# Token-major attend products in a single-core mLSTM and mixture-of-experts kernel

## What is computed

```python
for t in range(S):
    m_new = np.maximum(f_gate[:, :, t] + m, i_gate[:, :, t])
    f_stab = np.exp(f_gate[:, :, t] + m - m_new)
    i_stab = np.exp(i_gate[:, :, t] - m_new)
    m = m_new
    C = f_stab * C + i_stab * outer(v_t, k_t)
    n = f_stab * n + i_stab * k_t
    h = C @ q_t
    y[t] = sigmoid(o_gate_t) * h / max(|n . q_t|, 1)
```

## Time and profile before

| what | value |
|---|---|
| median of 3 runs | 378.28 us (377.2 to 378.36) |
| the profiled execution | 376.49 us |
| its span | 374.7 us |
| PE busy | 366.7 us, 98% |
| VectorE, ScalarE, GpSimd busy | 64%, 61%, 22% |
| granted PE clock | 1.0 throughout |

### The profile page before, as it was taken

One profiled execution on the slowest core, in us unless ns is written; L12 is line 12 of the kernel. 1 busy time (PEld: TensorE's weight loads), 2 busy tenths in 40 slices (PEclk: granted clock), 3 DMA queues, 4 the chain that ended last, 5 costly groups with the idle time before them and its releaser, 6 DMA issues.

```text
span 374.7 us, 9643 instructions
## 1 busy us (share of the span) xinstructions
PE 366.7 (98%) x3502; PEld 309.6 (83%) x3502; DVE 239.0 (64%) x576; ACT 229.9 (61%) x468; POOL 81.4 (22%) x124
## 2 busy tenths in 40 slices
PE   8999999999999999999999999999999999999996
PEld 6688777778777775354899999999999999999996
DVE  8778688468767864423877655565565556556553
ACT  4677776757667763120877666576666566666652
POOL 6674665447446540000000000000000000000000
PEclk9999999999999999999999999999999999999999
DMA  2869999999988979999100010010010001001002
GB/s 79 247 185 295 263 262 294 251 225 277 256 232 267 282 245 339 362 295 344 67 1 2 18 54 1 3 70 0 0 70 0 0 0 70 0 0 70 2 0 70
DMA packets 28792, 51.49 MB, mean 137 GB/s; under 512 B 2980, under 2 KB 20228, under 8 KB 28756
## 3 DMA queue, kind: packets, MB, share of 16 engines
q1 hardware_dynamic: 25388, 40.08, 36.4%
q10 hardware_dynamic: 3368, 10.93, 10.4%
HBM read 46.59 MB, written 4.33 MB: 136 GB/s over the span
## 4 chain that ended last, share of the span: by engine, by line
PE 92%; DMA 2%; ACT 2%; SPq 1%; issue 1%; DVE 1%; POOL 0%; ACTq 0%; POOLq 0%
PE heads_banks L1346 8%; PE heads_banks L1348 8%; PE heads_banks L1347 7%; PE high_banks L1347 7%; PE high_banks L1346 7%; PE high_banks L1348 7%; PE low_banks L959 6%; PE low_banks L1326 6%; PE heads_banks L980 5%; PE heads_banks L973 3%; PE high_banks L995 3%; PE low_banks L1014 3%; PE low_banks L939 3%; PE low_banks L1246 2%; PE high_banks L1005 2%; PE low_banks L1036 2%
## 5 line engine op out<-in xcount | busy, mean ns | idle before, releaser
L876 ACT ACTIVATE relu_h<-low_banks 128x512 f32<-128x512 f32 x94 | 56.3, 599 | 59.6 <-PE low_banks L1326 59.2
L1760 DVE CAST sq_hi<-sq_h 128x512 fp32r<-128x512 f32 x94 | 40.2, 427 | 64.1 <-ACT sq_h L881 63.5
L1762 DVE TENSOR_TENSOR sq_lo<-sq_h,sq_hi 128x512 fp32r<-128x512 f32 x94 | 65.1, 692 | 3.2
L881 ACT ACTIVATE sq_h<-relu_h 128x512 f32<-128x512 f32 x94 | 59.4, 632 | 3.0
L1346 PE MATMUL heads_banks<-wo_hi,sq_hi 128*128 128x320 f32 x192 | 59.3, 309 | 0.2 <-DVE sq_lo L1748 0.2
L1347 PE MATMUL high_banks<-wo_lo,sq_hi 128*128 128x320 f32 x192 | 59.4, 310 | 0.0
L1348 PE MATMUL high_banks<-wo_hi,sq_lo 128*128 128x320 f32 x192 | 59.4, 310 | 0.0
L1346 PE MATMUL high_banks<-wo_hi,sq_hi 128*128 128x320 f32 x192 | 59.4, 309 | 0.0
L1348 PE MATMUL heads_banks<-wo_hi,sq_lo 128*128 128x320 f32 x192 | 59.3, 309 | 0.0
L1347 PE MATMUL heads_banks<-wo_lo,sq_hi 128*128 128x320 f32 x192 | 59.3, 309 | 0.0
L1392 DVE TENSOR_TENSOR att_w<-low_banks,att_w 128x512 f32<-128x512 f32 x48 | 30.9, 685 | 25.4 <-PE low_banks L959 25.4
(11 more groups left out here) (217 smaller groups left out, 562.3 us busy)
## 6 DMA issues: line engine op xcount, KB each, us to landing
w_sb<-in_w SPq DMA_DIRECT2D x8, 1280.0 KB, 12.4
w_a<-in_w ACTq DMA_DIRECT2D x16, 512.0 KB, 7.0
kv_in<-in_kv SPq DMA_DIRECT2D x24, 320.0 KB, 8.6
qk_in<-in_qk SPq DMA_DIRECT2D x24, 256.0 KB, 4.8
o_in<-in_o_gate SPq DMA_DIRECT2D x24, 160.0 KB, 8.5
out<-out_sb SPq DMA_DIRECT2D x5, 640.0 KB, 3.2
wo_raw<-in_w_out SPq DMA_DIRECT2D x4, 640.0 KB, 11.5
w_b<-in_w ACTq DMA_DIRECT2D x8, 256.0 KB, 8.7
```

Of the source, the lines that this page charges most:

```text
L876: act.activation(relu_h[:, slot], bank[slot][:, :], ACT.Relu).then_inc(relu_done, 1)
L881: act.activation(sq_h[:, slot], relu_h[:, slot], ACT.Square).then_inc(sq_done, 1)
L1760: dve.tensor_copy(sq_hi[:, slot], sq_h[:, slot]).then_inc(hi_done, 1)
L1762: dve.tensor_tensor(sq_lo[:, slot], sq_h[:, slot], sq_hi[:, slot].bitcast(F32), ALU.subtract).then_inc(lo_done, 1)
```

## The change

The operands of the attend products change places. In the values part the masked weights (128 by 128) are loaded as weights and the values with their column of ones (41 columns) move; in the carried part the faded queries of two heads (128 by 128) are weights and the carried state moves. The heads so come out with tokens on partitions. The carried state is kept in blocks of two heads (`[P, 2, HP, 2, D + 1]`): both heads of a place j share the product, with zeros where a head's partitions meet the other head's columns, so that one product of 82 columns serves two heads. Two banks take turns for the heads, where one held them feature by feature in two halves and another their transposes. `copy_heads` and `turn_heads` go, and their semaphores. VectorE reads the denominators and heads from the attend bank; it updates the carried state ahead of the denominators, with an add for each half of the partitions. One clearing of `v_one` goes, and the one of `carry` grows with its tile.

```diff
-            carry = sb("carry", [P, 2, HP, DP], stack=own)
-            carry_faded = sb("carry_faded", [P, HP, D + 1], stack=own)
-            headsT = sb("headsT", [P, 2, 2, L], stack=own)
+            carry = sb("carry", [P, 2, HP, 2, D + 1], stack=own)
+            carry_faded = sb("carry_faded", [P, HP, 2, D + 1], stack=own)
...
-        heads_ps = heads_banks[:, :, 0:2 * L].rearrange("p o (i t) -> p o i t", i=2)
-        turned_ps = turned_bank[:, :].rearrange("p (j a e) -> p j a e", j=HP, a=2)
+        heads_ps = [own[:, :].rearrange("p (j a e) -> p j a e", j=HP, a=2) for own in (heads_bank, odd_bank)]
...
+        def place_of(j):
+            return 2 * (j % 2) + j // 2
+
+        def own_blocks(tile, r):
+
+            halves = tile[DP * r:DP * (r + 1)].rearrange("p (i t) a e -> p i (t a) e", i=2)
+            return halves[:, :, (slice(0, 4, 3), slice(1, 3))[r]]
...
-            sp.wait_ge(carry_ready, (NC - 1) * B)
+            sp.wait_ge(carry_ready, 2 * (NC - 1) * B)
...
             def weigh_keys(b, c):
...
-                at_least(pool, heads_turned, step(b, c) - 1)
+                at_least(pool, state_added, carries(b, max(c - 1, 0)))
...
-            pool.memset(v_one[:, :, :, D + 1:DP], 0.0).then_inc(v_cleared, 1)
...
             def copy_v(b, c):
...
-                at_least(act, heads_turned, step(b, c) - 1)
+                at_least(act, heads, step(b, c) - 1)
+                if (b, c) == (0, 2):
+                    act.wait_ge(state_added, 1)
...
-            def copy_heads(b, c):
-                act.wait_ge(heads, step(b, c) + 1)
-                at_least(act, heads_turned, step(b, c))
-                act.activation(headsT[:, :, :, :], heads_ps, ACT.Copy).then_inc(heads_out, 1)
...
             def attend(b, c):
 
                 s = c % 2
-                at_least(pe, heads_out, step(b, c))
+                to = heads_ps[step(b, c) % 2]
+                at_least(pe, norm_step, 4 * (step(b, c) - 2) + 3)
                 if c > 0:
                     pe.wait_ge(q_scaled, rescales(b, c))
-                    pe.wait_ge(carry_ready, carries(b, c))
+                    pe.wait_ge(carry_ready, 2 * carries(b, c))
                     for j in range(HP):
-                        for r in range(2):
-                            rows, a = slice(DP * r, DP * (r + 1)), half_of(r, j)
-                            pe.matmul(heads_ps[DP * a:DP * (a + 1), j % 2, j // 2], carry[rows, (c - 1) % 2, j], q_fade[rows, s, j],
-                                      start=j < 2, stop=False, skip_group_check=True)
+                        pe.matmul(to[:, place_of(j), :, 0:D + 1], q_fade[:, s, j], carry[:, (c - 1) % 2, j],
+                                  start=j == 0, stop=False, skip_group_check=True)
                 pe.wait_ge(weights, step(b, c) + 1)
                 pe.wait_ge(v_ready, step(b, c) + 1)
                 for j in range(HP):
                     for r in range(2):
-                        h, a = HP * r + j, half_of(r, j)
-                        mm = pe.matmul(heads_ps[DP * a:DP * (a + 1), j % 2, j // 2], v_one[:, s, h], att_w[:, s, h],
-                                       start=c == 0 and j < 2, stop=True, skip_group_check=True)
+                        h = HP * r + j
+                        mm = pe.matmul(to[:, place_of(j), half_of(r, j), 0:D + 1], att_w[:, s, h], v_one[:, s, h, 0:D + 1],
+                                       start=c == 0 and h == 0, stop=True, skip_group_check=True)
                 mm.then_inc(heads, 1)
...
-            def turn_heads(b, c):
-                pe.wait_ge(heads_out, step(b, c) + 1)
-                at_least(pe, x_ready, step(b, c))
...
-                for j in range(HP):
-                    mm = pe.transpose(turned_bank[:, P * j:P * (j + 1)], headsT[:, j // 2, j % 2], ident)
-                mm.then_inc(heads_turned, 1)
...
             def update_carry(b, c):
-                dve.wait_ge(state_added, carries(b, c) + 1)
                 at_least(dve, heads, step(b, c))
+                fresh = state_ps[:, :, 0:D + 1].rearrange("p (i t) e -> p i t e", i=2)
...
                 dve.wait_ge(fade_ready, rescales(b, c))
-                whole = fade_b[:, fade_slot(b, c), :, L - 1].unsqueeze(2).broadcast_to([P, HP, D + 1])
-                dve.tensor_tensor(carry_faded[:, :, :], carry[:, (c - 1) % 2, :, 0:D + 1], whole, ALU.mult).then_inc(carry_half, 1)
+                dve.wait_ge(carry_ready, 2 * carries(b, c))
+                whole = fade_b[:, fade_slot(b, c), :, L - 1].unsqueeze(2).broadcast_to([P, HP, 2 * (D + 1)])
+                both = "p j a e -> p j (a e)"
+                dve.tensor_tensor(carry_faded.rearrange(both), carry[:, (c - 1) % 2].rearrange(both), whole, ALU.mult).then_inc(carry_half, 1)
                 dve.wait_ge(carry_half, (NC - 2) * b + c)
-                dve.tensor_tensor(carry[:, c % 2, :, 0:D + 1], carry_faded[:, :, :], state_ps[:, :, 0:D + 1], ALU.add)\
-                    .then_inc(carry_ready, 1)
+                dve.wait_ge(state_added, carries(b, c) + 1)
+                for r in range(2):
+                    dve.tensor_tensor(own_blocks(carry[:, c % 2], r), own_blocks(carry_faded, r), fresh[DP * r:DP * (r + 1)], ALU.add)\
+                        .then_inc(carry_ready, 1)
...
             def denominators(b, c):
 
                 n = step(b, c)
-                dve.wait_ge(heads_turned, n + 1)
+                own_heads = heads_ps[n % 2]
+                dve.wait_ge(heads, n + 1)
+                at_least(dve, x_ready, n)
...
             def vec_step(b, c, half, nxt=True, cur=True, prev=True, rb=None):
+                if cur and c < NC - 1:
+                    update_carry(b, c)
                 if prev:
                     denominators(*before(b, c))
-                if cur and c < NC - 1:
-                    update_carry(b, c)
```

More of the change, by code:

```diff
@@ L341, in build_program @@
         decay_bank, score_bank = bank[0:2], bank[2:4]
-        merge_bank, heads_bank, turned_bank, side_bank = bank[4], bank[5], bank[6], bank[7]
-        heads_ps = heads_banks[:, :, 0:2 * L].rearrange("p o (i t) -> p o i t", i=2)
-        turned_ps = turned_bank[:, :].rearrange("p (j a e) -> p j a e", j=HP, a=2)
+        merge_bank, heads_bank, odd_bank, side_bank = bank[4], bank[5], bank[6], bank[7]
+        heads_ps = [own[:, :].rearrange("p (j a e) -> p j a e", j=HP, a=2) for own in (heads_bank, odd_bank)]
         state_ps = side_bank[:, 0:HP * DP].rearrange("p (j e) -> p j e", j=HP)
@@ L352, in build_program @@
         last_turn = bank[3][:, 0:NC * NS].rearrange("p (c s) -> p c s", c=NC)
[L353 removed]
+        late_turn = merge_bank[:, 0:NC * NS].rearrange("p (c s) -> p c s", c=NC)
         turn_ps = side_bank[:, 0:NC * NS].rearrange("p (c s) -> p c s", c=NC)
@@ L781, in _ @@
             src_high(1)
-            act.wait_ge(v_cleared, 2)
+            act.wait_ge(v_cleared, 1)
             copy_v(0, 0)
@@ L793, in act_step @@
                     raise_keyw(1)
[L794 to L797, removed]
+                if cur and c < NC - 1:
+                    raise_fade(b, c + 1)
                 if rb is not None and c == NC - 1 and b < B - 1:
@@ L988, in add_state @@
                 pe.wait_ge(v_ready, step(b, c) + 1)
-                at_least(pe, carry_ready, carries(b, c))
+                at_least(pe, carry_ready, 2 * carries(b, c))
                 if rb is not None:
@@ L1141, in pe_step @@
                     if cur and c > 0:
-                        pe.wait_ge(carry_ready, carries(b, min(c + 1, NC - 1)))
+                        pe.wait_ge(carry_ready, 2 * carries(b, min(c + 1, NC - 1)))
                     route(rb, c, 1 - half)
@@ L1212, in _ @@
             for k in range(KC):
-                mm = pe.matmul(turned_bank[0:P if k < 2 else DP, QUAD * k:QUAD * (k + 1)], slot_acc[:, P * k:min(P * (k + 1), DM)],
+                mm = pe.matmul(odd_bank[0:P if k < 2 else DP, QUAD * k:QUAD * (k + 1)], slot_acc[:, P * k:min(P * (k + 1), DM)],
                                fold_scaled[:, :], start=k == 0, stop=True, skip_group_check=True)
-            mm = pe.matmul(turned_bank[DP:P, 2 * QUAD:KC * QUAD], slot_acc[:, DM - DP:DM], fold_scaled[:, :],
+            mm = pe.matmul(odd_bank[DP:P, 2 * QUAD:KC * QUAD], slot_acc[:, DM - DP:DM], fold_scaled[:, :],
                            start=False, stop=True, skip_group_check=True)
@@ L1408, in denominators @@
             def denominators(b, c):
                 n = step(b, c)
-                dve.wait_ge(heads_turned, n + 1)
+                own_heads = heads_ps[n % 2]
+                dve.wait_ge(heads, n + 1)
+                at_least(dve, x_ready, n)
                 dve.wait_ge(gate_ready, n + 1)
                 halves = "p (j a) -> p j a"
-                dve.tensor_scalar(norm_neg[:, :].rearrange(halves, a=2), turned_ps[:, :, :, D], -2.0, 2.0,
+                dve.tensor_scalar(norm_neg[:, :].rearrange(halves, a=2), own_heads[:, :, :, D], -2.0, 2.0,
@@ L1419, in denominators @@
```

(2 more changed lines are left out.)

13 lines of the change are left out of this document (3 added, 10 removed).

## The result

| what | before | after |
|---|---|---|
| median of the runs side by side | 378.32 us (377.2 to 378.67, 4 runs) | 444.3 us (439.36 to 454.32, 4 runs) |
| the profiled execution, its span | 376.49, 374.7 | 446.29, 444.6 |
| mean granted PE clock in that span | 1.0 | 0.869 |
| the expert products start at | 162.8 us | 232.6 us |

The changed kernel takes 1.1658 times as long, 95% interval [1.1581, 1.1736]. The forecast was 398 us, 393 to 402. The four runs of the changed kernel differ more than those of before, and in the order of their granted clock: 439.36 us at 0.887, 442.31 at 0.88, 446.29 at 0.869, 454.32 at 0.849.

What follows compares the result with a forecast made beforehand. PE's issue rate was taken as the bound. Terms 23.0 - 1.1 + 1.8 + 0.1 - 2.2 - 1.3 = +20.3 us on the profiled 376.49 gave 396.8, stated as 398 us for the median, 8-in-10 range 393 to 402.

Steps and rivals of the forecast that it cites:

- Rival A: Attend products: a record's pace follows the moving columns, not the weights, so faster, 367 us; 4%.
- Rival B: Attend products: with wide weights the next load waits for the stream, 24 records take 3.76 us, 420 us total; 2%.
- Rival D: Attention steps: a new wait of 0.3 us a step for the faded queries, some 7 us in all, 405 us; 6%.
- Attend groups at 2.77 us: Carried and values products: 24 records at 0.11 plus 0.13 turn, against 1.62 before; +1.15 in 20 steps, +23.0.
- the first chunks: Three first chunks of later batches, no carried part: 1.89 us where 1.30 pass now, +0.59 each, +1.8.
- Heads transposes in ordinary steps: Removing them saves only 0.20 us in each of 11 steps, as PE then waits for x's copy: -2.2.
- rival C: x's copy never waited for, or small waits hide behind attend; the transposes' full 10 us come back, 391 us; 5%.
- Where logits follow: Seven steps with router logits: of the transposes' 0.44 us some 0.26 is given back, 0.18 saved each, -1.3.
- Chunk 4, nothing saved: In chunk 4 no state product follows and the chain is bare already, so removing the heads transposes saves nothing.
- The rest costs nothing: VectorE, ScalarE, GpSimd and SP work changed outside PE's groups adds no time; x's readiness has 2 us of cover.
- Sum: All terms together: 23.0 - 1.1 + 1.8 + 0.1 - 2.2 - 1.3 = +20.3 us.

Runs made afterwards that it cites:

- e1_pad: Changed kernel with both moving operands of attend zero-padded, 64 columns instead of 41 (values) and 128 instead of 82 (carried): 397.74 us.
- e10_padv_bank: Changed kernel with x's transposes in a bank of their own and the values part padded to 64 moving columns: 393.78 us.
- e3_split: Changed kernel with each attend product issued twice, for tokens 0 to 63 and 64 to 127, side by side in two column halves: 382.58 us.
- e6_bank_pad: e3_split with x's transposes in the bank free during attention and the values part padded to 64 moving columns: 382.47 us.
- e7_order: e6_bank_pad with SyncE issuing chunk 4's loads of queries, keys and values ahead of phi and the wait for stored rows: 381.58 us.
- e1c_padc: Changed kernel with only the carried part padded, 128 moving columns instead of 82; the values part moves 41: 404.51 us.

## Why the prediction was wrong

**The step that failed** is one that was taken without a sum. The prediction read a granted clock of 1.0 in every slice and used durations of before for everything that the change doesn't touch. So it put the clock at nothing without a reason: those durations hold only while the clock stays where it was. In the changed kernel 116 us of the span pass at 1.2 GHz. Of the 69.9 us of growth, e1_pad's span (396.1, clock 1.0) puts 21.4 on the groups and waits, and leaves the other 48.5 to the clock. The runs of the changed kernel say the same by themselves: from the fastest (span 437.6, clock 0.887, so 98.9 us at 1.2 GHz) to the slowest (452.6, 0.849, 136.7 us) 37.8 us more at the low clock cost 15.0 us, 0.40 each; 98.9 x 0.40 = 39 off 439.4 leaves 400, and e1_pad measures 397.7. No rival had such a mechanism: A and B were about a record's pace, D about waits. The range ended 37 us below the fastest run.

**The other steps, at full clock:**

- Attend groups at 2.77 us: 2.81 measured, 2.70 where a transpose follows (2.68 forecast), 1.91 in the first chunks (1.89 forecast). Right; with the measured values the term is 8 x 1.19 + 12 x 1.08 = 22.5, where 23.0 - 1.1 = 21.9 was forecast.
- Rival A, moving columns set the pace: refuted by the same numbers, and by 64 columns taking no longer than 41. Rival B, a load waits for the stream: refuted by the padded kernel, 0.99 and 1.83 at 128 and 64 columns.
- Heads transposes in ordinary steps, 0.20 each: 1.95 became 1.74. Right, and rival C, that x's copy is never waited for, is refuted with it.
- Where logits follow, 0.18 each: wrong, 0. The reckoning let the first 8 logit records run while the rest waits, and the group behind end sooner; it ends as late as before, 2.03 both. That is 1.3 us too much saved.
- Chunk 4, nothing saved: 1.22 before and after. Right.
- Rival D, 0.3 us a step for faded queries: refuted. The padded kernel has one such wait, 0.72 us in the last batch's chunk 4, where there was one before; the changed one has none. "The rest costs nothing" holds for VectorE, ScalarE and GpSimd: the only wait that the list names from 15 to 190 us is the forecast one on x's copy, 2.0 us in 3. The 0.84 us on VectorE ahead of the first values product is outside it; e1_pad has no such wait and e10_padv_bank one of 0.81.
- Sum: +22.5 + 1.8 + 0.1 - 2.3 = +22.1 by these measured terms, and +21.4 in e1_pad's span; +20.3 was forecast. So the sum was right to about 2 us for a kernel that keeps the clock. That 398 meets e1_pad's 397.74 so closely is in part luck: two terms were off by 0.6 and 1.3 us, and by medians e1_pad lies 19.4 us above the kernel before, by spans 21.4.

**What set the clock.** Shown: padding both operands is enough to hold it, with all waits in place; with the waits away, padding the values alone is enough; taking the waits away without padding gives most of it back (0.869 to 0.958 in the profiled runs) and fillers do too (0.975); the old products with similar short waits keep 1.0 in the profiled run. So thin streams and short waits both count, and they add. In the kernels with halves the clock falls at longer idle time: within a wait of 1.09 us in e3_split, and within 1 us of the end of waits of 3.39 and 1.78 in e6_bank_pad and 2.90 in e7_order, where padding the values didn't prevent it. That these waits cause those falls is only argued: e7_order took one away and got another. Not settled: what exactly starts a fall. The first one comes at 16.8 us in the changed kernel, at 62.7 us in the one with the own bank. The wait of 0.84 us shortly before the first doesn't explain it: e1c_padc falls at 16.5 us, behind one of 0.17, and e10_padv_bank has 0.81 there and doesn't fall. One kernel's runs also differ in how long they pass at 1.2 GHz (clocks of 0.919 and 0.958 with the own bank).
The Trainium skill ("TensorE: Matmul & The Clock Gate", Part 1) says that the clock follows how busy PE has been, and warns of idle gaps. Here PE was busy 40.00 of 40.00 us by the trace at a clock of 0.57, and no gap in its steps was over 0.84 us, in that stretch none; the measurement decides: a busy share near 100% doesn't warrant the full clock.

## What to carry to other kernels

Before a product's operands are swapped, reckon both the pace (a record goes by the wider of weights and moving columns, so keep 64-column tiles side by side) and how few columns will stream behind each load; if they become few, treat the clock of all PE work around as at risk and price it at the other level as a rival. A cheap test is to pad the moving operand with zeros: if the kernel gets faster, look for the clock. And transposes that look like pure cost may stand in the shadow of a copy, so removing them earns only what is left once the next wait is reached.

## What the runs showed of the hardware that was not expected

- The granted clock fell to 1.2 GHz for 116 us in a kernel whose PE is busy 98% of the span, as busy as before. Streaming 23 zero columns more per values record and 46 more per carried record made it 46.6 us faster.
- At 1.2 GHz nearly all PE groups take 1.7 to 1.9 times as long: the carried part 1.79 against 0.96, the state product 1.01 against 0.59, the decay 0.72 against 0.43. The short waits of ordinary steps for other engines are hidden then (that of 0.67 in chunk 4 is not, at 156.88 us), so a fallen clock makes PE look better fed.
- The kernel before is itself near the edge: of its 19 runs beside the first experiments, 11 had a clock of 0.999 or 1.0 (376.19 to 378.61 us) and 8 one of 0.990 to 0.995 (378.5 to 382.04 us). A few per mille between two runs of one kernel can be the clock.
